# Merging the scores of two key blocks with a predicated copy, in the attention stage of a fused attention, mixture-of-experts and MLP kernel

## The chip, the core and the metric

The kernel runs on one core of a Trainium2 chip. The metric is the device time of one execution in microseconds (us). The core has five engines, each with an instruction stream of its own that runs in order: TensorE (PE in the profile; its weight loads are shown apart as PEld), VectorE (DVE), ScalarE (ACT), GpSimd (POOL) and SyncE (SP), which here only issues DMAs. The streams meet at semaphores: an instruction adds to one when it has finished, and another stream waits until it has reached a value.

## The reference

The batch is 4, there are 8 heads, 768 positions and 64 numbers per head. Attention keeps, for each position, the first 4 keys (the sinks) and the last 128 keys up to itself:

```python
scores = scale * np.matmul(q, k.transpose(0, 1, 3, 2))
keep = is_sink | in_window          # key < 4, or 0 <= query - key < 128
scores = np.where(keep, scores, -1e9)
a = np.exp(scores - max); a = a / (sum(a) + 1e-9)
attn = np.matmul(a, v)
x = attn as rows (3072, 512)
# mixture of experts: rows with x @ w_skip > 0 get the one expert of 8 with the largest gate logit
h = np.maximum(xc[mask] @ w1[e], 0); y[mask] = gate_w[mask, None] * (h @ w2[e]); out = x + y
# MLP on all rows
return np.maximum(x @ w_in, 0) ** 2 @ w_out
```

## The kernel before

Attention works on 24 tiles of 128 positions (`TILES`, six to a batch). A window of 128 keys that ends at the position itself lies in two blocks of keys: the tile's own block and the block before it. For a query in row r the own block gives keys 0 to r, and the block before gives the keys behind r: each column of the two blocks is wanted from one of them only, never from both. The first tile of a batch (`is_first`: tiles 0, 11, 17 and 23 in the order of work) has its own block alone. Each block is held with the 4 sinks in front, so it is `KB` = 132 columns wide.

For one tile i the stages are these. `scores(i, heads)` on PE multiplies queries and keys of a head into one of four PSUM banks (`SCORE_BANKS`), 264 columns wide (132 on a first tile); head n waits until the maximum of head n-4 has freed its bank. `maximum(i, h)` on DVE (L1190) reads a bank, adds a mask, scales and writes the scores and the row's negative maximum. `exps` on ACT (L667) makes the weights `prob`. `turn(i, k)` on PE (L897) turns the weights of a pair of heads k, four pieces of 128 x 128, and one `turn` for the sinks of all heads; `turned` on ACT (L680) copies them out of PSUM. `product(i, k)` on PE (L924) multiplies turned weights and values, own block and block before, into `oT_ps`. `take_output` (L1313, on DVE) copies `oT_ps` to `xT_a`, `logits` (L949) and `rows_back` (L935) on PE make the router's logits and turn the output back, `logits_back` turns the logits after DVE's `take_logits` (L1327), `normalise` on DVE (L1304) divides by the sum. DVE's `abreast` cuts the routing into pieces of tiny instructions (`choose`, `place`), one piece in front of each maximum. GpSimd splits the sink weights into two parts (`prob_sink`, L583 and L585) and scatters finished rows (L594).

The order on each engine is written out by hand, as a loop over steps i in which several tiles are at work. On PE step i is: turns 2, 3 and sinks of tile i-1; `scores(i, 4..7)`; four products of i-1; `logits` and `rows_back` of i-2; `turn(i, 0)`; ranks of i-3; `logits_back(i-2)`; `scores(i+1, 0..3)`; `turn(i, 1)`; the sink product of i-1. On DVE it is: `take_output(i-2)`; maxima 4 to 7 of tile i with routing pieces; sums; `take_logits` and `normalise` of i-2; reciprocals; maxima 0 to 3 of tile i+1, a routing piece in front of each. In steps 13 to 20 ACT also makes the upper half of the first expert's weights, and in steps 14 to 21 DVE the lower (L340, two a step).

Of the kernel before, what the change touches and what calls it, by code (L numbers as in the profile page):

```python
# [47 lines left out]
SINK = PAIRS  # L48
ITEMS = PAIRS + 1
# [26 lines left out]
def build(nc, n_sink, window, qT, kT, v, v_sink, w_route, weights, out):  # L76
# [10 lines left out]
    with ctx:  # L87
# [15 lines left out]
        masks = sb("masks", [P, 5, 2, KB], F32, big)  # L103
# [5 lines left out]
        score = sb("score", [P, 2, H, 2 * KB], F32, big)  # L109
        prob = sb("prob", [P, 2, H, 2 * KB], F32, big)  # L110
        prob_sink = sb("prob_sink", [P, 2, 2, H, NS], F32R, big)
        probT = sb("probT", [P, PAIRS, 4 * P], F32, big)
# [80 lines left out]
        bank = [ctx.enter_context(nc.psum_tensor(f"bank{n}", [P, 512], F32)) for n in range(8)]  # L193
# [20 lines left out]
        s_turn, s_turned, s_pv = sem("s_turn"), sem("s_turned"), sem("s_pv")  # L214
        s_xT, s_back = sem("s_xT"), sem("s_back")
# [34 lines left out]
        MASK_KINDS = ((1, 1, NS), (3, 1, 0), (4, 0, 0), (2, 0, NS))  # L250
        MASKS_MADE = (1, 3, 9, 5, 7)
# [45 lines left out]
        def mask_kind(i):  # L297

            return 0 if is_first(i) else {1: 2, 2: 4}[min(ORDER[i][1], 2)] - own_at(i)

        def width(i):

            return KB * len(blocks(i))
# [242 lines left out]
        def _(eng):  # L546
# [3 lines left out]
            def keep_up_to(part, first):  # L550

                eng.affine_select(out=part, in_=part, compare_op=ALU.is_ge, fill=out_of, base=-first, pattern=[[-1, P - first]], channel_multiplier=1)\
                   .then_inc(s_mask, 1)

            def keep_after(part, first):

                eng.affine_select(out=part, in_=part, compare_op=ALU.is_gt, fill=out_of, base=first, pattern=[[1, P - first]], channel_multiplier=-1)\
                   .then_inc(s_mask, 1)

            keep_up_to(masks[:, 0, 0, 2 * NS:KB], NS)  # L560
            eng.affine_select(out=ident[:, :], in_=ident[:, :], compare_op=ALU.not_equal, fill=1.0, base=0, pattern=[[-1, P]], channel_multiplier=1)\
               .then_inc(s_ident, 1)
            for kind, own, first in MASK_KINDS:
                keep_up_to(masks[:, kind, own, NS:KB], 0)
                keep_after(masks[:, kind, 1 - own, NS + first:KB], first)
# [11 lines left out]
            for i in range(TILES + 3):  # L577
                if i < TILES:
                    eng.wait_ge(s_exp, H * (i + 1))
                    if i >= 1:  # L580
                        eng.wait_ge(s_turn, ITEMS * i)
                    sinks = prob[:, i % 2, :, KB * own_at(i):KB * own_at(i) + NS].rearrange("p (v h) k -> p v h k", v=1).to_broadcast([P, 2, H, NS])
                    eng.tensor_copy(prob_sink[:, :, 0, :, :], sinks).then_inc(s_pshi, 1)  # L583
                    eng.wait_ge(s_pshi, i + 1)
                    eng.tensor_tensor(prob_sink[:, :, 1, :, :], sinks, prob_sink[:, :, 0, :, :].bitcast(F32), ALU.subtract).then_inc(s_psink, 1)  # L585
                j = i - 3
                if j < 0:
                    continue
                n = j % XR
                eng.wait_ge(s_slot, j + 1)  # L590
                if j == EARLY:
# [4 lines left out]
                   .then_inc(s_scatter[n], 16)  # L596

# [53 lines left out]
        def _(eng):  # L651
# [5 lines left out]
            def exps(i, heads):  # L657

                for h in heads:
# [7 lines left out]
                    eng.activation(prob[:, i % 2, h, 0:width(i)], score[:, i % 2, h, 0:width(i)], ACT.Exp, bias=neg_max[:, i % 2, h:h + 1],  # L667
                                   scale=-1.0, accum_out=row_sum[:, i % 2, h:h + 1]).then_inc(s_exp, 1)

            def turned(i, k):  # L670

                eng.wait_ge(s_turn, ITEMS * i + k + 1)
                if i >= 1:

                    eng.wait_ge(s_pv, ITEMS * (i - 1) + k + 1)
                if k == SINK:
                    eng.activation(sinkT[:, :], route_ps[:, SINKS:SINKS + P], ACT.Copy).then_inc(s_turned, 1)
                else:
                    cols = 2 * P * len(blocks(i))
                    eng.activation(probT[:, k, 0:cols], turn_ps[k % 2][:, 0:cols], ACT.Copy).then_inc(s_turned, 1)  # L680
# [21 lines left out]
            for i in range(TILES + 1):  # L702
# [9 lines left out]
                if bb:  # L712
                    turned(i - 1, 2)
                if a:
                    exps(i, (2,))
                if bb:
                    turned(i - 1, 3)
                    turned(i - 1, SINK)
                if a:
                    exps(i, (3,))  # L720
# [130 lines left out]
        def _(eng):  # L851
# [3 lines left out]
            def scores(i, heads):  # L855

                at = blocks(i)
                for h in heads:
# [10 lines left out]
                    eng.matmul(score_ps[n % SCORE_BANKS][:, 0:width(i)], q_in[rows, i % 3, h // 2, :], keys, start=True, stop=True).then_inc(s_score, 1)  # L869

            def turn(i, k):

                to = turn_ps[k % 2]
# [9 lines left out]
                else:  # L883
                    eng.wait_ge(s_exp, H * i + 2 * k + 2)

                    if k >= 2:
                        eng.wait_ge(s_turned, ITEMS * i + k - 1)
                    elif k == 0 and i >= 1:
                        eng.wait_ge(s_turned, ITEMS * i - 2)
                    elif k == 1 and i >= 2:  # L890
                        eng.wait_ge(s_x, i - 1)
                    elif k == 1 and i == 1:
                        eng.wait_ge(s_turned, ITEMS * i - 1)
                    u = 0
                    for half in range(2):
                        for at in range(len(blocks(i))):
                            ins = eng.transpose(to[:, u * P:(u + 1) * P], prob[:, i % 2, 2 * k + half, at * KB + NS:(at + 1) * KB], ident[:, :])  # L897
                            u += 1
                ins.then_inc(s_turn, 1)

            def product(i, k):
# [3 lines left out]
                eng.wait_ge(s_turned, ITEMS * i + k + 1)  # L905
                at = blocks(i)
# [674 lines left out]
```

## Time and profile before

| | us |
|---|---|
| median of 3 runs | 922.82 (922.46 to 923.65) |
| the profiled execution | 924.29 |
| its span, first to last instruction | 922.8 |
| of it attention, up to the drain of the last tile | about 190 |
| PE busy in the span | 899.4 (97%) |
| DVE, ACT, POOL busy | 473.3, 421.4, 81.7 |

"Busy" counts the time in which an engine has at least one instruction at work. The chain of waits is followed back from the last instruction: at each step to what released it, or to the instruction before it on its engine. A piece of it is therefore time that the end of the kernel has depended on. A timeline row gives start, duration, engine, line and operation, what it writes and reads, and in brackets how long the engine had been idle and what it then waited for.

### The profile page before, as it was taken

The numbers are of one execution on the slowest core, as the hardware profiler recorded it, in microseconds if no ns is written. First come the engines' busy times: TensorE is split into PE (matmuls) and PEld (weight loads), VectorE is DVE, ScalarE is ACT, GpSimd is POOL, SyncE is SP. The second block draws the span as 40 slices with busy tenths as digits, with TensorE's granted clock in tenths as the row PEclk, the third lists the DMA queues.
The fourth block names the chain that finished last, engine by engine and source line by source line (L and its number), as shares of the span: only waits on it lengthen the run. The fifth ranks groups of instructions, "written<-read, shape, count | busy, mean of one in ns | idle before, by whom it ended". The sixth has DMA issues, their size and how long they took to land.

```text
span 922.8 us, 16992 instructions
## 1 busy us (share of the span) xinstructions
PE 899.4 (97%) x5152; PEld 730.2 (79%) x5153; DVE 473.3 (51%) x1419; ACT 421.4 (46%) x970; POOL 81.7 (9%) x147
## 2 busy tenths in 40 slices
PE   7999999989999998999999999999999999999998
PEld 5778777757888886878888888888888888888886
DVE  5787899886776667764242224222422342243224
ACT  7888899835666666553132113221312231232123
POOL 3112121223111111100000000000000000000000
PEclk9999999999999999999999999999999999999999
DMA  5556675285667678740003002100400040004001
GB/s 200 170 160 201 225 239 173 71 296 186 240 248 250 245 245 311 242 106 0 1 36 57 1 1 67 24 0 0 91 0 0 0 91 0 0 0 91 0 0 45
DMA packets 87364, 99.52 MB, mean 108 GB/s; under 512 B 56093, under 2 KB 56221, under 8 KB 87312
## 3 DMA queue, kind: packets, MB, share of 16 engines
q1 hardware_dynamic: 81168, 83.34, 28.6%
q0 software_dynamic: 6000, 15.49, 4.9%
q8 instruction: 25, 0.41, 0.2%
q14 instruction: 27, 0.22, 0.1%
q10 hardware_dynamic: 144, 0.07, 0.0%
HBM read 77.72 MB, written 25.56 MB: 112 GB/s over the span
## 4 chain that ended last, share of the span: by engine, by line
PE 91%; issue 2%; ACT 2%; DMA 2%; DVE 2%; ACTq 1%; DVEq 0%; SPq 0%; POOLq 0%
PE bank L1128 28%; PE bank L1114 28%; PE bank L1029 7%; PE bank L1010 7%; PE bank L869 5%; PE bank L924 4%; PE bank L897 4%; PE bank L935 1%; PE bank L1018 1%; PE bank L949 1%; PE bank L917 1%; DMA w_raw<-in_weights 1%; PE bank L1002 1%; ACT prob L667 0%; DVE x_row L1304 0%
## 5 line engine op out<-in xcount | busy, mean ns | idle before, releaser
L1498 DVE TENSOR_TENSOR g<-relu_c 128x512 f32<-128x512 f32 x96 | 66.4, 692 | 340.7 <-ACT relu_c L812 340.7
L812 ACT ACTIVATE relu_c<-bank 128x512 f32<-128x512 f32 x96 | 57.4, 598 | 371.7 <-PE bank L1114 371.7
L1114 PE MATMUL bank<-x_hi,w_lo 128*128 128x512 f32 x384 | 149.5, 389 | 0.7 <-DVE x_lo L1485 0.7
L1128 PE MATMUL bank<-w_hi,g_lo 128*128 128x512 f32 x384 | 150.1, 391 | 0.0
L1128 PE MATMUL bank<-w_hi,g_hi 128*128 128x512 f32 x384 | 149.4, 389 | 0.0
L1128 PE MATMUL bank<-w_lo,g_hi 128*128 128x512 f32 x384 | 149.4, 389 | 0.0
L1114 PE MATMUL bank<-x_lo,w_hi 128*128 128x512 f32 x384 | 149.4, 389 | 0.0
L1114 PE MATMUL bank<-x_hi,w_hi 128*128 128x512 f32 x384 | 149.4, 389 | 0.0
L667 ACT ACTIVATE prob<-score,neg_max 128x264 f32<-128x264 f32 (+1 forms) x192 | 94.0, 496 | 15.2 <-DVE neg_max L1190 15.2
L1457 DVE TENSOR_TENSOR w_lo<-w_raw,w_hi x70 | 82.0, 1221 | 21.2 <-issue 13.3
L1128 PEld LDWEIGHTS bank<-w_hi,g_lo 128*128 128x128 f32 x384 | 72.1, 188 | 17.3 <-DVE g_lo L1505 2.5
L1114 PEld LDWEIGHTS bank<-x_hi,w_lo 128*128 128x128 f32 x384 | 72.1, 188 | 16.1 <-DVE x_lo L1485 1.2
L1128 PEld LDWEIGHTS bank<-w_hi,g_hi 128*128 128x128 f32 x384 | 72.1, 188 | 15.0
L1114 PEld LDWEIGHTS bank<-x_hi,w_hi 128*128 128x128 f32 x384 | 72.1, 188 | 15.0
L1114 PEld LDWEIGHTS bank<-x_lo,w_hi 128*128 128x128 f32 x384 | 72.1, 188 | 15.0
L1128 PEld LDWEIGHTS bank<-w_lo,g_hi 128*128 128x128 f32 x384 | 72.1, 188 | 14.8
L1190 DVE CUSTOM_DVE_ANT_0 score<-bank,masks 128x264 f32<-128x264 f32 (+1 forms) x192 | 74.4, 403 | 13.7 <-PE bank L869 5.3
L775 ACT ACTIVATE w_hi<-w_raw x70 | 69.5, 1050 | 18.7 <-DVE w_lo L1457 10.4
L1505 DVE TENSOR_TENSOR g_lo<-g,g_hi 128x512 fp32r<-128x512 f32 x96 | 65.6, 684 | 0.0
L821 ACT ACTIVATE g_hi<-g 128x512 fp32r<-128x512 f32 x96 | 60.0, 625 | 4.1 <-PE bank L1128 4.1
L869 PE MATMUL bank<-k_in,q_in 64*128 64x264 f32 (+1 forms) x384 | 54.9, 403 | 5.4 <-DMA k_in<-in_kT 5.4
L897 PE MATMUL bank<-ident,prob 128*128 128x128 f32 x352 | 56.0, 283 | 3.5 <-ACT probT L680 2.9
(149 smaller groups left out, 1280.3 us busy)
## 6 DMA issues: line engine op xcount, KB each, us to landing
w_raw<-in_weights SPq DMA_DIRECT2D x80, 512.0 KB, 4.9
k_in<-in_kT SPq DMA_DIRECT2D x24, 264.0 KB
q_in<-in_qT SPq DMA_DIRECT2D x24, 256.0 KB, 3.4
v_in<-in_v SPq DMA_DIRECT2D x24, 256.0 KB
x_rows<-x_row SPq DMA_DIRECT2D x24, 256.0 KB, 3.3
x_row<-x_rows SPq DMA_DIRECT2D x96, 64.0 KB, 2.4
out<-w_raw SPq DMA_DIRECT2D x12, 512.0 KB, 2.9
x_res<-routed POOLq DMA_DIRECT2D x15, 260.0 KB, 3.4
```

The source lines that it names most:

```text
L667: eng.activation(prob[:, i % 2, h, 0:width(i)], score[:, i % 2, h, 0:width(i)], ACT.Exp, bias=neg_max[:, i % 2, h:h + 1], scale=-1.0, accu ...
L775: eng.activation(w_hi[1 - slot][:, f, :], w_raw[:, f, :], ACT.Copy).then_inc(s_whi, 1)
L869: eng.matmul(score_ps[n % SCORE_BANKS][:, 0:width(i)], q_in[rows, i % 3, h // 2, :], keys, start=True, stop=True).then_inc(s_score, 1)
L897: ins = eng.transpose(to[:, u * P:(u + 1) * P], prob[:, i % 2, 2 * k + half, at * KB + NS:(at + 1) * KB], ident[:, :])
L1010: ins = eng.matmul(h_ps[half][:, :], x[:, c, :], w[:, c, cols], start=(c == 0 and k == 0), stop=(c == DC - 1 and k == 2))
L1029: ins = eng.matmul(y_ps[:, :], h[:, c // 4, at], w[:, DC + c // 2, cols], start=(c == 0 and k == 0), stop=(c == FC - 1 and k == 2))
L1114: ins = eng.matmul(hc_ps[f % 2][:, :], w[f // UNIT][:, f % UNIT, wcols], x[:, c, :], start=(c == 0 and n == 0), stop=(c == DC - 1 and n == 2))
L1128: ins = eng.matmul(yc_ps[s][:, :], gg[:, f % 2, s * P:(s + 1) * P], w[f // UNIT][:, f % UNIT, DM:CH], start=(f == 0 and n == 0), stop=(f = ...
L1190: eng.tensor_tensor_reduce(score[:, i % 2, h, 0:width(i)], score_ps[n % SCORE_BANKS][:, 0:width(i)], masks[:, mask_kind(i), 0:len(blocks(i ...
L1457: eng.tensor_tensor(w_lo[1 - slot][:, f, :], w_raw[:, f, :], w_hi[1 - slot][:, f, :].bitcast(F32), ALU.subtract).then_inc(s_wlo, 1)
L1498: eng.tensor_tensor(g[:, f % 2, :], relu_c[:, f % 2, :], relu_c[:, f % 2, :], ALU.mult).then_inc(s_cg, 1)
L1505: eng.tensor_tensor(g_lo[:, f % 2, :], g[:, f % 2, :], g_hi[:, f % 2, :].bitcast(F32), ALU.subtract).then_inc(s_cglo, 1)
```

## The change

Two scores of a column are never both wanted, so one instruction on DVE, `merge(i, k)`, copies the block before over the own block in PSUM where the column lies behind the query, for four heads (all four banks) at once. From there on a head has 132 columns instead of 264: the maximum, the exponential and the scores' and weights' buffers. PE turns four pieces for four heads instead of eight, and ACT copies them out in one instruction per four heads. The products still need own block and block before apart, so GpSimd splits the turned weights with two selections per four heads (`split`): one writes `probT_own`, the other clears `probT` in place. `take_output` moves from DVE to ACT within the loop. PE's order changes: the turn of heads 4 to 7 now lies at the start of the next step, and the products are two, the second behind `rows_back`. GpSimd's scatter of a tile moves one turn of its loop later. `quad` is the four score banks as one tensor. The masks are fewer, and first tiles are neither merged nor split.

```diff
 # GpSimd
+def split(i, k):
+    if is_first(i): return
+    eng.wait_ge(s_turned, ITEMS * i + k + 1)
+    eng.affine_select(out=probT_own[:, k, :, :], in_=probT[:, k, :, :], compare_op=ALU.is_ge, fill=0.0, base=0,
+                      pattern=[[0, QUAD], [1, P]], channel_multiplier=-1).then_inc(s_split, 1)
+    eng.affine_select(out=probT[:, k, :, :], in_=probT[:, k, :, :], compare_op=ALU.is_gt, fill=0.0, base=0,
+                      pattern=[[0, QUAD], [-1, P]], channel_multiplier=1).then_inc(s_split, 1)
-for i in range(TILES + 3):
+for i in range(TILES + 4):
+    if 1 <= i <= TILES: split(i - 1, 1)
+    if i >= 4: scatter(i - 4)
     ...
+        split(i, 0)
 # ScalarE, step i
-    exps(i, (1,)); turned(i - 1, 2); exps(i, (2,)); turned(i - 1, 3); turned(i - 1, SINK); exps(i, (3,))
+    exps(i, (1,)); turned(i - 1, SINK); take_output(i - 2); exps(i, (2, 3))
 # TensorE
-    eng.wait_ge(s_turned, ITEMS * i + k + 1)
+    if k == SINK or is_first(i): eng.wait_ge(s_turned, ITEMS * i + k + 1)
+    else: eng.wait_ge(s_split, SPLITS * others(i) + 2 * k + 2)
     ...
-                    turn(i - 1, 2)
-                    turn(i - 1, 3)
+                    turn(i - 1, 1)
                     turn(i - 1, SINK)
                 if a:
                     scores(i, (4, 5, 6, 7))
                 if bb:
-                    for k in range(PAIRS):
-                        product(i - 1, k)
+                    product(i - 1, 0)
                 if c:
                     logits(i - 2)
                     rows_back(i - 2)
+                if bb:
+                    product(i - 1, 1)
                 if a:
                     turn(i, 0)
     ...
-                if a:
-                    turn(i, 1)
 # VectorE
+def merge(i, k):
+    eng.wait_ge(s_score, H * i + QUAD * (k + 1))
+    if is_first(i): return
+    own, other = (slice(at * KB + NS, at * KB + KB) for at in (own_at(i), 1 - own_at(i)))
+    eng.copy_predicated(quad[:, :, own], later_keys[:, :, :].bitcast(I32), quad[:, :, other]).then_inc(s_merged, 1)
 def maximum(i, h):
-    eng.wait_ge(s_score, n + 1)
+    if h % QUAD == 0 and not is_first(i):
+        eng.wait_ge(s_merged, QUADS * others(i) + h // QUAD + 1)
     ...
-                if c:
-                    take_output(i - 2)
+                if a:
+                    merge(i, 1)
     ...
                 if i + 1 < TILES:
+                    merge(i + 1, 0)
                     for h in range(4):
                         next(routing, None)
                         maximum(i + 1, h)
```

## Rows read from the trace of the kernel before

**Rows 1.** Busy time in a stretch: PE, PEld, DVE, ACT, POOL, granted clock, DMA share, GB/s

```profile
100.00:120.00 20.00, 20.00 (x207) 15.70 (x209) 17.71 (x105) 18.90 (x62) 4.53 (x9) 1.00 0.70 234
```

**Rows 2.** Chain that ended last, one step: start, us, engine and line

```profile
103.18 1.09 PE bank L869 x8
104.27 1.90 PE bank L924 x32
106.17 0.36 PE bank L949 x8
106.52 0.59 PE bank L935 x4
...
107.75 1.09 PE bank L869 x8
108.84 0.59 PE bank L897 x4
...
109.83 1.01 PE bank L897 x8
...
110.94 1.09 PE bank L869 x8
```

**Rows 3.** Same chain: the turn of the sinks in steps 3 and 23

```profile
26.07 0.11 PE bank L882
...
180.26 0.11 PE bank L882
```

**Rows 4.** Groups by line and form: count, busy us, mean ns, idle before

```profile
L667 ACT ACTIVATE prob<-score,neg_max 128x264 f32<-128x264 f32 x160 | 81.3, 515 | 12.1 <-DVE neg_max L1190 12.1
L1190 DVE CUSTOM_DVE_ANT_0 score<-bank,masks 128x264 f32<-128x264 f32 x160 | 65.9, 426 | 10.0 <-PE bank L869 5.1 <-DVE slot_i L1264 3.4
L680 ACT ACTIVATE probT<-bank 128x512 f32<-128x512 f32 x80 | 47.3, 591 | 4.7 <-PE bank L897 4.7
L1313 DVE COPY xT_a<-bank 128x512 f32<-128x512 f32 x24 | 16.5, 686 | 0.2
L1190 DVE CUSTOM_DVE_ANT_0 score<-bank,masks 128x132 f32<-128x132 f32 x32 | 8.5, 288 | 3.7 <-issue 2.8 <-DVE slot_i L1264 0.6 <-PE bank L869 0.3
L552 POOL TENSOR_SCALAR_AFFINE_SELECT masks<-masks 128x128 f32<-128x128 f32 x4 | 1.1, 282 | 0.0
```

**Rows 5.** Chain, step 1: four scores on PE

```profile
12.61 1.09 PE bank L869 x8
```

**Rows 6.** Timeline of DVE, step 1: the first maximum of those four heads

```profile
13.29 0.43 DVE L1190 CUSTOM_DVE_ANT_0 score<-bank,masks 128x264 f32<-128x264 f32 x1 [1.64 <-PE bank L869]
```

**Rows 7.** Timeline of DVE: a routing piece in front of the first maximum

```profile
100.16 0.18 DVE L1199 TENSOR_TENSOR head_logit<-bank,recip 128x72 f32<-128x72 f32 x1
...
100.41 0.14 DVE L1243 TENSOR_SCALAR expsum_eps<-expsum 128x1 f32<-128x1 f32 x1
```

**Rows 8.** Timeline of DVE, step 18: first and fourth maximum, then two copies

```profile
139.75 0.42 DVE L1190 CUSTOM_DVE_ANT_0 score<-bank,masks 128x264 f32<-128x264 f32 x1
...
141.87 0.43 DVE L1190 CUSTOM_DVE_ANT_0 score<-bank,masks 128x264 f32<-128x264 f32 x1 [0.20 <-DVE slot_i L1264]
...
142.22 0.69 DVE L1313 COPY xT_a<-bank 128x512 f32<-128x512 f32 x1
142.83 0.68 DVE L340 TENSOR_TENSOR w_lo<-w_raw,w_hi 128x512 fp32r<-128x512 f32 x1
```

**Rows 9.** Chain, step 18: the products behind scores that waited for those maxima

```profile
143.07 1.08 PE bank L924 x16
```

**Rows 10.** Timeline of DVE: maxima 4 to 7 with routing, first and next

```profile
103.77 0.15 DVE L1222 TENSOR_REDUCE best<-cand 128x1 f32<-128x8 f32 x1
...
105.54 0.17 DVE L1290 TENSOR_SCALAR sum_eps<-row_sum 128x8 f32<-128x8 f32 x1
```

**Rows 11.** Busy time by stretch as in Rows 1: the drain of attention

```profile
184.00:193.00 9.00, 6.15 (x68) 4.50 (x66) 7.02 (x40) 2.65 (x8) 1.32 (x2) 1.00 0.95 322
193.00:196.00 3.00, 2.72 (x9) 1.70 (x10) 1.93 (x12) 0.39 (x2) 0.98 (x1) 0.52 1.03 416
```

More of the change, by code:

```diff
@@ L297, in mask_kind, with others @@
         def mask_kind(i):
-            return 0 if is_first(i) else {1: 2, 2: 4}[min(ORDER[i][1], 2)] - own_at(i)
-        def width(i):
-            return KB * len(blocks(i))
+            return min(ORDER[i][1], LATER)
+        def others(i):
+            return sum(not is_first(n) for n in range(i))
         def step_flags(i):
@@ L883, in turn @@
                 else:
[L884 to L889, printed above, removed]
+                    eng.wait_ge(s_exp, H * i + QUAD * (k + 1))
+                    if k == 0 and i >= 1:
+                        eng.wait_ge(s_turned, ITEMS * (i - 1) + 1)
                     elif k == 1 and i >= 2:
@@ L892, in turn @@
                     elif k == 1 and i == 1:
[L893 to L898, printed above, removed]
+                        eng.wait_ge(s_turned, 2)
+                    for u in range(QUAD):
+                        ins = eng.transpose(to[:, u * P:(u + 1) * P], prob[:, i % 2, QUAD * k + u, NS:KB], ident[:, :])
                 ins.then_inc(s_turn, 1)
             def product(i, k):
-                eng.wait_ge(s_turned, ITEMS * i + k + 1)
-                at = blocks(i)
+                if k == SINK or is_first(i):
+                    eng.wait_ge(s_turned, ITEMS * i + k + 1)
+                else:
+                    eng.wait_ge(s_split, SPLITS * others(i) + 2 * k + 2)
                 if k == 0:
@@ L919, in product @@
                 else:
-                    for n, ring in enumerate(at):
-                        for half in range(2):
-                            h = 2 * k + half
-                            u = half * len(at) + n
-                            ins = eng.matmul(oT_ps[half * D:(half + 1) * D, k * P:(k + 1) * P], v_in[:, ring, h * D:(h + 1) * D],
-                                             probT[:, k, u * P:(u + 1) * P],
-                                             start=(k == 0 and n == 0), stop=False, skip_group_check=True)
+                    own = own_load(i) % RING, probT if is_first(i) else probT_own
+                    parts = [own] if is_first(i) else [own, (before_load(i) % RING, probT)]
+                    for p in range(QUAD // 2):
+                        for n, (ring, part) in enumerate(parts):
+                            for half in range(2):
+                                u = 2 * p + half
+                                h = QUAD * k + u
+                                ins = eng.matmul(oT_ps[half * D:(half + 1) * D, h // 2 * P:(h // 2 + 1) * P], v_in[:, ring, h * D:(h + 1) * D],
+                                                 part[:, k, u, :], start=(k == 0 and p == 0 and n == 0), stop=False, skip_group_check=True)
                 ins.then_inc(s_pv, 1)
@@ L1074, in expert @@
                     tile(n, slot, parts)
-            turn(TILES - 1, 2)
-            turn(TILES - 1, 3)
+            turn(TILES - 1, 1)
             turn(TILES - 1, SINK)
-            for k in range(PAIRS):
+            for k in range(QUADS):
                 product(TILES - 1, k)
```

116 lines of the change are left out of this document (64 added, 52 removed).

## The prediction, made before the changed kernel was run

> **What bounds the kernel now.** I read the busy table by stretch first. In attention PE is busy for all of 20 us, ACT for 18.90 and DVE for 17.71, at full granted clock [rows 1]: three engines near their limit, so the table doesn't say which one a change is worth something on. The chain of waits does: through most of attention it runs piece after piece on PE with no wait between, and the step repeats after 7.76 us (the scores of heads 4 to 7 at 103.18 and at 110.94) [rows 2]. From the sinks' turn in step 3 to that in step 23 twenty steps take 154.2 us, 7.71 each [rows 3]. Nothing behind attention is touched but the places in the code and 8 buffers, so the forecast is a sum over these steps.
>
> **PE's work.** The change takes away eight of the sixteen turns, the piece of 1.01 us [rows 2]. All other matmuls stay: scores are still 264 wide on PE, and the products still need own block and block before. Alone, PE would need 7.76 - 1.01 = 6.75 us a step. The question is whether it is kept fed.
>
> **The new round trip.** Call T0 the end of the scores of heads 0 to 3 of a tile, T1 the end of those of heads 4 to 7. Both groups use the same four banks. Before, the first maximum began as soon as the first pair of heads had landed. Now the merge waits for all four heads, and the first maximum for the merge; and it stands ahead of the routing piece on DVE, which used to run while the scores were under way. Between T0 and T1 PE has only the sink product, four turns and the sinks' turn: 110.94 - 108.84 = 2.10, less the 1.01 that goes: 1.09 us; before the change the 2.10 just covered the maxima. From T0 to T1 the steps are now:
> - PE to DVE: a group took 1.09 us [rows 5], and its first maximum came 13.29 - 12.61 = 0.68 us after its start [rows 6]. That is the first pair, half the group; the last pair is 0.545 later, 0.14 behind the group's end.
> - The merge: no row shows a predicated copy, nor DVE writing PSUM. The nearest is the copy of 128x512 out of PSUM, 686 ns [rows 4], 0.61 from its start to the next instruction's [rows 8]. It has as many columns; I take 0.61. Below it I see no gain, since it reads a mask besides; above, twice as much, 1.22.
> - The routing piece in front of the first maximum: 0.25 from its first to its last start [rows 7], with an estimated 0.06 for the last 0.31.
> - The four maxima with the other routing pieces, and the last score. In step 18 of before PE did wait for these maxima: the first started at 139.75, the fourth at 141.87 [rows 8], and the work behind the last score at 143.07 [rows 9]. That is 3.32 us. Each maximum gets shorter by 426 - 288 = 138 ns [rows 4], four by 0.55: 2.77.
>
> The sum is 0.14 + 0.61 + 0.31 + 2.77 = 3.83 us. PE has 1.09 of other work and 1.09 of scores to put into it, so it stands still for 1.65 us.
>
> **The rest of the step** holds the same instructions as before, in another order: from 104.27 (products) to 108.84 (end of the next scores) 4.57 us [rows 2]. The second merge and maxima 4 to 7 lie under this: 0.14 + 0.61 + (105.54 - 103.77 - 0.55 = 1.22) [rows 10] is 2.0, and the next scores are asked for after 3.5. A step is then 3.83 + 4.57 = 8.40 us, against 7.71.
>
> **The other parts.** ACT loses two of four copies of 591 ns and 132 of 264 columns of eight exponentials of 515 ns [rows 4]; it gains the output copy. It is not in the round trip, but PE's products at T1 wait for that copy now: first maximum, an exponential, a copy, another exponential, the sinks and the output copy end about 3.6 us behind T0, so just hidden under 3.83; if that cover goes it costs some tenths a step. DVE loses 8 x 0.138 and the output copy, 0.61, and gains two merges, 1.22: about 0.5 less, and it waits for PE anyway. GpSimd gains four selections a step. One over 128 columns took 282 ns [rows 4]; over 512 it lies between that and four times as much, 1.13. I take the upper end, as the work is by column. Four are 4.5 us, on top of 4.53 / 20 x 7.76 = 1.76 [rows 1], of a step of 8.4. The splits of heads 4 to 7 begin at T0 + 2.5 and end by 4.8; their product is asked for at T1 + 0.95 + 0.36 + 0.59 [rows 2], T0 + 5.7. So they are hidden, and would bind from about 1.6 us each. The scatter moves one turn of GpSimd's loop, behind two waiting splits; the row buffer that it frees is wanted two steps later, and at the end of attention it can delay the first expert tile's load once, by two selections at most, 2.3 us; I cost it at nothing, for the drain is full of other waits.
>
> In steps 14 to 21 DVE also makes the weights' lower halves, 0.61 each as spaced [rows 8]. Then `take_logits` ends at T1 + 0.14 + 0.61 + 0.61 + 1.22 + 0.10 + 0.61 + 0.35 = 3.64, and PE wants its result about 0.3 earlier: 0.3 more in each of these eight steps.
>
> **The sum.** Twenty steps at 8.40 are 168.0. Add 8 x 0.3 = 2.4. Where the batch changes I take off, by estimate, 0.44 three times (narrow scores), 0.95 once (half the products) and 0.83 twice (no merge): 3.9. That is 166.5 against 154.2: +12.3. Steps 1 and 2 have little or no routing, and there the 1.01 comes through about once: -1.0. Net +11.3 us. The profiled execution took 924.29 (span 922.8 and 1.5 around it), so it would go to 935.6; the median of the runs was 922.82, 1.5 lower, and goes to **934.1 us**.
>
> **Rival: PE stays the bound.** Then a step is 6.75 and twenty save 20 us: 903. For that the round trip must be 2.18 or less. Already merge and four bare maxima, 0.14 + 0.61 + 4 x 0.29 = 1.9, and the last score, at least a quarter of 1.09, come to that. The point at which the kernel stops losing is a round trip of 3.83 - 11.3 / 20 = 3.26, so if some 0.6 us of the routing vanished beside the maxima, of about 1.3 (0.31, and what the 2.12 holds beside three maxima, 0.85 to 1.0). For it speaks that these instructions overlap a little; against it that each piece waits for the one before, and that the 3.32 is measured with the overlap in it. About 912, chance 0.08; another 0.06 for no change, 921 to 924.7.
>
> **Rival: GpSimd holds up DVE.** The second pair of splits begins at T0 + 2.5, and just then DVE runs the last routing piece in front of the fourth maximum. If the two engines got in each other's way there, a routing instruction would wait for up to one selection, 0.28 to 1.13; at 0.6 this is 12 us more, 946. The Trainium skill says that it is so (SBUF — State Buffer, "Who interferes with whom"): a DVE instruction with two inputs in SBUF and a GpSimd instruction that reads SBUF exclude each other for the length of one; two instructions of that piece, `cand` and `slot_i`, have two such inputs. No row here shows it, as GpSimd is busy for a quarter of the time [rows 1] and elsewhere. A merge of 1.22 would give the same size: +12. Together 0.28.
>
> **Rival: the clock falls.** In the drain PE was busy for 6.15 of 9 us, 68%, and then the granted clock was 0.52, the lower level (1.2 GHz) [rows 11]. A step of 6.75 in 8.40 is 80%. If half the steps ran their 4.57 at the lower clock, they would take 10 x 4.57 = 46 us more: 980. Chance 0.06, as the stall is broken up by four scores.
>
> **How the numbers follow.** The forecast as summed, 925 to 940, has 0.52. Faster by over 0.2% (about what a measurement of this kernel can tell from no change) has 0.08, within 0.2% 0.06, slower 0.52 + 0.28 + 0.06 = 0.86. The range goes from 924 to 952: it takes in the forecast and the rival with GpSimd or a dear merge, and leaves out the faster case, most of no change, and the clock.
>
> **What would show it.** In the profile after, PE should be idle for some 1.6 us a step in front of the scores of heads 4 to 7, the wait ending on DVE's negative maximum, and the chain should go through merge, maxima and routing pieces. The piece of turns should be gone, the products as long as before. The merge should take about 0.69 us, a selection under 1.13. I am wrong if PE's chain is still unbroken, if a step is under 7.7 us, or if PE waits in front of the products for GpSimd or ACT instead.

## The result and the profile after

The changed kernel takes 947.63 us (946.52 to 948.08), the kernel before beside it 923.15: a ratio of 1.0264, 95% interval 1.0246 to 1.0282. That is 24.5 us slower where 11.3 had been forecast; the sign and the range held, but the forecast was less than half of what came. The profiled spans differ by 22.7 us (945.5 and 922.8).

The busy line of the page after (engine, busy us, share of the span, instructions):

```profile
PE 918.5 (97%) x4992; PEld 727.0 (77%) x4993; DVE 464.3 (49%) x1427; ACT 396.5 (42%) x944; POOL 130.4 (14%) x221
```

PE looks full, and is not. The ends of matmuls are modelled in the profile, and the modelled lengths of the scores cover most of the waits between their banks: from 115.01 to 118.77 us PE counts as busy for 3.65 of 3.76 us. The chain shows the wait. One step of the changed kernel, to be read against [rows 2] (start us, us, what):

```profile
115.01 0.02 issue
115.03 0.70 DVE quad L1205
115.73 0.09 DVE head_logit L1225
...
116.01 0.26 DVE score L1216
...
117.70 0.30 DVE score L1216
...
118.06 0.71 PE quad L891 x2
118.77 1.02 PE bank L946 x16
119.79 0.35 PE bank L970 x8
120.15 0.59 PE bank L956 x4
120.74 1.02 PE bank L946 x16
121.76 0.59 PE bank L915 x4
...
122.55 1.14 PE quad L891 x8
123.69 0.02 issue
123.71 0.70 DVE quad L1205
```

The chain leaves PE for 3 us in an ordinary step: T0 is at 115.01, then merge, routing pieces and maxima on DVE, and only the last head's scores bring it back; T1 is at 118.77. The step is 8.68 us long, where [rows 2] has 7.76.

What the parts cost, from the groups by form up to the first expert tile (busy us, mean ns of one | idle before):

```profile
L1205 DVE COPY_PREDICATED quad<-later_keys,quad 128x512 f32<-128x512 int32 x40 | 27.8, 696 | 46.7 <-PE quad L891 46.7
L1216 DVE CUSTOM_DVE_ANT_0 score<-quad,masks 128x132 f32<-128x132 f32 x192 | 52.3, 287 | 9.1 <-DVE slot_i L1290 4.0 <-issue 3.8 <-PE quad L891 0.9
L685 ACT ACTIVATE prob<-score,neg_max 128x132 f32<-128x132 f32 x192 | 75.7, 397 | 56.1 <-DVE neg_max L1216 54.7 <-issue 1.5
L585 POOL TENSOR_SCALAR_AFFINE_SELECT probT_own<-probT 128x512 f32<-128x512 f32 x40 | 25.6, 640 | 43.4 <-ACT probT L697 43.4
```

The merge is the 0.69 that was named, a maximum 287 ns against the 426 of [rows 4], and a selection 0.64, well under the 1.13 taken for it. ACT, at 18.90 of 20 us before [rows 1], now has 56 us of idle time in front of its exponentials, nearly all of it waiting for DVE's maxima.

Where the 22.7 us of the span lie, by the start of the sinks' turn in each tile (tiles 2 and 22 are at 25.91 and 180.10 before, at 30.34 and 202.16 after; the first expert matmul at 192.90 and 216.68):

| stretch | forecast | measured |
|---|---|---|
| to tile 2 | -1.0 | +4.4 |
| tile 2 to tile 22, twenty steps | +12.3 | +17.6 |
| tile 22 to the first expert matmul | 0 | +1.7 |
| behind it | 0 | -1.1 |

### The profile page after: what moved, and what is told of

Read it like the earlier page. It is cut to its first block, busy times and chain, and to the rows that moved or that the text cites. A ratio compares the mean times of both kernels' runs of the same rounds, so it can differ in the third digit from the quotient of the medians.

```text
span 945.5 us, 16614 instructions
## 1 busy us (share of the span) xinstructions
PE 918.5 (97%) x4992; PEld 727.0 (77%) x4993; DVE 464.3 (49%) x1427; ACT 396.5 (42%) x944; POOL 130.4 (14%) x221
## 4 chain that ended last, share of the span: by engine, by line
PE 86%; DVE 7%; issue 3%; DMA 1%; ACT 1%; ACTq 1%; DVEq 0%; SPq 0%; POOLq 0%
PE bank L1146 28%; PE quad L1132 28%; PE bank L1048 7%; PE quad L1029 7%; PE bank L946 5%; PE quad L891 5%; DVE score L1216 2%; PE bank L915 2%; DVE quad L1205 1%; PE bank L956 1%; PE bank L970 1%; PE quad L1021 1%; PE quad L1037 1%; DMA w_raw<-in_weights 1%; PE bank L1037 1%
## 5 line engine op out<-in xcount | busy, mean ns | idle before, releaser
L834 ACT ACTIVATE relu_c<-quad 128x512 f32<-128x512 f32 x96 | 57.4, 598 | 371.6 <-PE quad L1132 371.6
L1132 PE MATMUL quad<-x_hi,w_lo 128*128 128x512 f32 x384 | 149.5, 389 | 0.7 <-DVE x_lo L1513 0.7
L1132 PE MATMUL quad<-x_hi,w_hi 128*128 128x512 f32 x384 | 149.4, 389 | 0.0
L1132 PE MATMUL quad<-x_lo,w_hi 128*128 128x512 f32 x384 | 149.4, 389 | 0.0
L685 ACT ACTIVATE prob<-score,neg_max 128x132 f32<-128x132 f32 x192 | 75.7, 397 | 56.1 <-DVE neg_max L1216 54.7
L891 PE MATMUL quad<-k_in,q_in 64*128 64x264 f32 (+1 forms) x384 | 79.7, 420 | 9.7 <-DMA k_in<-in_kT 5.5
L1132 PEld LDWEIGHTS quad<-x_hi,w_lo 128*128 128x128 f32 x384 | 72.1, 188 | 16.1 <-DVE x_lo L1513 1.1
L1132 PEld LDWEIGHTS quad<-x_hi,w_hi 128*128 128x128 f32 x384 | 72.1, 188 | 15.0
L1132 PEld LDWEIGHTS quad<-x_lo,w_hi 128*128 128x128 f32 x384 | 72.1, 188 | 14.9
L797 ACT ACTIVATE w_hi<-w_raw x70 | 69.6, 1051 | 17.6 <-DVE w_lo L1485 9.4
L1216 DVE CUSTOM_DVE_ANT_0 score<-quad,masks 128x132 f32<-128x132 f32 x192 | 52.3, 287 | 9.1 <-DVE slot_i L1290 4.0
```

Of the source, the lines that this page charges most:

```text
L685: eng.activation(prob[:, i % 2, h, :], score[:, i % 2, h, :], ACT.Exp, bias=neg_max[:, i % 2, h:h + 1], scale=-1.0, accum_out=row_sum[:, i ...
L797: eng.activation(w_hi[1 - slot][:, f, :], w_raw[:, f, :], ACT.Copy).then_inc(s_whi, 1)
L891: eng.matmul(score_ps[n % SCORE_BANKS][:, 0:KB * len(at)], q_in[rows, i % 3, h // 2, :], keys, start=True, stop=True).then_inc(s_score, 1)
L1132: ins = eng.matmul(hc_ps[f % 2][:, :], w[f // UNIT][:, f % UNIT, wcols], x[:, c, :], start=(c == 0 and n == 0), stop=(c == DC - 1 and n == 2))
L1216: eng.tensor_tensor_reduce(score[:, i % 2, h, :], score_ps[h % QUAD][:, own_at(i) * KB:own_at(i) * KB + KB], masks[:, mask_kind(i), :], -S ...
```

## The experiments

Theory: in each step PE stands still in a round trip through DVE over the four banks, as forecast; on top of it come single terms of the sum that were mis-sized. Rivals: GpSimd's selections hold up DVE or the products; the clock. Two more questions came from the table: the start, and the seams between kinds of work on PE. The table gives every kernel tried. The ratio is to the kernel before as run beside each, whose median lay between 923.15 and 925.02, so medians of two rows compare to within some 2 us. The columns behind it are read from the start of the sinks' turns in the one profile of each kernel: where tile 2 begins, the step from tile 6 to 7 (an ordinary one), from 10 to 11 (tile 11 is a batch's first tile), and from 19 to 20 (DVE makes weights' halves); then the first expert matmul.

| kernel | median us | ratio to before (95%) | tile 2 | 6-7 | 10-11 | 19-20 | expert |
|---|---|---|---|---|---|---|---|
| before | 923.15 | | 25.91 | 7.76 | 7.50 | 7.76 | 192.90 |
| after | 947.63 | 1.0246-1.0282 | 30.34 | 8.67 | 10.30 | 8.75 | 216.68 |
| e1_product_later | 933.69 | 1.0066-1.0126 | 28.10 | 7.65 | 7.65 | 8.76 | 201.58 |
| e2_piece_first | 944.69 | 1.0192-1.0248 | 29.68 | 8.60 | 9.90 | 8.67 | 214.59 |
| e3_both | 932.07 | 1.0056-1.0111 | 28.01 | 7.66 | 7.66 | 8.69 | 201.25 |
| e4_no_splits | 949.74 | 1.0250-1.0314 | 27.86 | 8.66 | 8.20 | 8.74 | 211.08 |
| e6_copy_twice | 980.50 | 1.0566-1.0641 | 33.01 | 9.41 | 9.48 | 10.22 | 252.21 |
| e7_start | 943.80 | 1.0183-1.0252 | 27.07 | 8.67 | 8.75 | 8.75 | 211.84 |
| e8_pieces_behind | 941.53 | 1.0150-1.0221 | 28.28 | 8.45 | 8.20 | 8.45 | 208.34 |
| e9_pieces_act | 930.42 | 1.0055-1.0103 | 29.16 | 7.61 | 7.16 | 8.32 | 196.02 |
| e10_act | 943.68 | 1.0197-1.0250 | 27.52 | 8.67 | 8.31 | 8.75 | 211.00 |
| e11_dense_start | 944.77 | 1.0199-1.0256 | 26.69 | 8.67 | 8.76 | 8.75 | 211.45 |
| e12_sparse_start | 946.12 | 1.0206-1.0279 | 29.06 | 8.67 | 8.75 | 8.75 | 216.88 |
| e13_seam | 944.85 | 1.0186-1.0235 | 30.37 | 8.63 | 8.16 | 8.75 | 213.48 |
| v4_all | 923.24 | 0.9976-1.0011 | 28.11 | 7.12 | 6.53 | 8.30 | 191.72 |
| v5_halves | 917.86 | 0.9910-0.9945 | 26.47 | 7.12 | 6.53 | 7.68 | 183.82 |
| v6_start | 917.05 | 0.9896-0.9952 | 26.67 | 7.12 | 6.53 | 7.67 | 184.17 |

### Work for the round trip

```
                     rows_back(i - 2)
-                if bb:
-                    product(i - 1, 1)
...
                 if bb:
+                    product(i - 1, 1)
                     product(i - 1, SINK)
```

> The products of heads 4 to 7 of the tile before are moved behind the scores of heads 0 to 3 of the next tile, on PE alone; all else is the changed kernel. Theory (round trip through DVE over the four banks): the piece of 1.02 us moves out of the chain behind the second scores (4.92 to 3.90 us) into the stall, where PE stands still for about 1.6 us; the round trip stays at 3.76, a full step goes from 8.67 to about 7.7 us and the time by about 20 us, to 925 to 932. Rival (GpSimd's selections hold up DVE or the products) and rival (the clock): the amount of each engine's work is the same, so a step stays at about 8.6 and the time at 944 to 950.

An ordinary step fell from 8.67 to 7.65, the 1.02 of the moved piece to a hundredth; the rivals, by which it would have stayed at about 8.6, are out for ordinary steps. The time, 933.69, missed the 925 to 932: most steps in which DVE makes weights' halves stayed near 8.76. Their chain (start us, us, what) and the end of their queue on DVE (start us, us, instruction):

```profile
167.35 0.44 PE bank L915 x4
167.78 0.94 issue
168.73 0.17 PE bank L985
```
```profile
167.74 0.69 DVE L348 TENSOR_TENSOR w_lo<-w_raw,w_hi 128x512 fp32r<-128x512 f32 x1
168.34 0.28 DVE L1353 COPY lgT<-bank 128x128 f32<-128x128 f32 x1
```

PE stands 0.94 us in front of the ranks, which wait for the logits' copy, and that copy is queued on DVE behind a weights' half. The round trip is not the only loop there.

### The parts of the round trip

e6_copy_twice makes each merge twice, the second behind the first:

```
+                eng.copy_predicated(quad[:, :, own], later_keys[:, :, :].bitcast(I32), quad[:, :, other]).then_inc(s_again, 1)
+                eng.wait_ge(s_again, QUADS * others(i) + k + 1)
                 eng.copy_predicated(quad[:, :, own], later_keys[:, :, :].bitcast(I32), quad[:, :, other]).then_inc(s_merged, 1)
```

> Each merge of the changed kernel is made twice, the second copy behind the end of the first (the second changes nothing in the scores). Theory (round trip through DVE): the copy in front of heads 0 to 3 lies in the round trip, 0.70 us and up to 0.17 for the wait behind it, in twenty steps: 14 to 17 us more, 961 to 966; the copy in front of heads 4 to 7 stays hidden. Rival (the time is lost where PE's products wait for GpSimd or ACT, or at the clock; DVE has some 2.9 us of slack in a step): 0 to 4 us more, 947 to 952.

The ordinary step rose by 0.74, from 8.67 to 9.41: the merge ahead of heads 0 to 3 lies wholly on the path. The time rose by 33, twice what was expected. In the steps with weights' halves both merges count, by the size of the rise (10.22 against 8.75), and six steps took 10.9 to 12.5, with the granted clock down in five of them. A stretch in one of these (us, PE busy, PEld, DVE, ACT, POOL, granted clock, DMA share, GB/s):

```profile
86.00:88.00 2.00, 2.00 (x16) 1.45 (x16) 1.31 (x3) 0.78 (x6) 1.01 (x1) 0.50 0.17 26
```

0.50 is the lower level, 1.2 GHz; from 82 to 84 us, at 1.00, PE had been busy for 1.22 of 2.00 us. So the rival with the clock is real, at a longer stall than the change makes.

```
+                    next(routing, None)
                     merge(i + 1, 0)
                     for h in range(4):
-                        next(routing, None)
+                        if h:
+                            next(routing, None)
                         maximum(i + 1, h)
```

> On DVE the first routing piece is put back in front of the first merge of a tile, so that it runs while the scores of heads 0 to 3 are under way. Theory (round trip): about 0.3 us leaves the round trip in each of some twenty steps: 940 to 943. Rival (GpSimd) and rival (clock): 946 to 949.

The step fell by 0.07, not 0.3. With the piece gone, DVE stands idle for 0.17 us between the merge and the first maximum, which waits for the merge's end; the routing piece had been running in that gap (timeline of DVE, idle time and its releaser in brackets):

```profile
62.75 0.29 DVE L1216 CUSTOM_DVE_ANT_0 score<-quad,masks 128x132 f32<-128x132 f32 x1 [0.17 <-DVE quad L1205]
```

e3_both has both edits:

> Both edits: the products of heads 4 to 7 behind the next tile's first scores on PE, and the first routing piece ahead of the first merge on DVE. Theory (round trip): 3.45 us of round trip hold 1.09 + 1.02 + 1.14 = 3.25 us of PE's work, 3.90 stand outside: a step of about 7.35 us, and the time near 919 to 925, about that of the kernel before. Rivals: above 940.

7.66 and 932.07, no less than e1 alone and above what was expected: something else ends as late as DVE's loop. The next two kernels name it.

```
                     merge(i + 1, 0)
+                    next(routing, None)
                     for h in range(4):
-                        next(routing, None)
                         maximum(i + 1, h)
+                    for _ in range(3):
+                        next(routing, None)
```

> On DVE the second, third and fourth routing pieces stand behind the four maxima of heads 0 to 3 instead of between them; all else is the changed kernel. Theory (round trip): these pieces lie in the round trip, about 0.75 us: a full step goes from 8.67 to about 7.9 us, a little less in the steps with the weights' halves, and the time to 931 to 937. Rival (routing instructions overlap the maxima or PE's other work anyway) and rival (GpSimd, clock): 944 to 949.

Only 0.22 a step. The products at T1 now wait for ACT's output copy, and no longer for DVE (timelines of PE and ACT, idle time and its releaser in brackets):

```profile
73.59 0.44 PE L946 MATMUL bank<-probT_own,v_in 128*64 128x128 f32 x4 [0.77 <-ACT xT_a L705]
```
```profile
72.86 0.59 ACT L705 ACTIVATE xT_a<-bank 128x512 f32<-128x512 f32 x1
```

The products begin 3.47 us behind T0 (70.12), where the prediction has "about 3.6" for the end of that copy. In e3's chain it is the same copy (67.49 to 68.09, its products at 68.23): there the moved product stands ahead of PE's turn of heads 4 to 7, and so of all that ACT does behind it. e10 makes that copy earlier on ACT, in the changed kernel, and e9 does so in e8:

```
                     exps(i, (0,))
+                if a and c:
+                    take_output(i - 2)
                 if bb:
                     turned(i - 1, 1)
...
-                if a and c:
-                    take_output(i - 2)
```

> The changed kernel with the output copy ahead of the copy of the second turned weights on ACT, nothing else. Theory (DVE's loop of 3.76 us ends last in the changed kernel, ACT's is hidden under it): no change, 945 to 949. Rival (the products' wait for the output copy is what limits the changed kernel): 0.2 us and more a step, 943 or below.

> The changed kernel with the second to fourth routing pieces behind the four maxima on DVE and, besides, the output copy on ACT ahead of the copy of the second turned weights. Theory (two loops of nearly the same length between the two groups of scores: DVE's with merge and maxima, 3.76 us, and ACT's with exponential, two copies and the output copy, about 3.5): with both shortened the round trip is DVE's without the pieces, about 3.0, and a full step 7.9 to 8.0 us where DVE makes no halves of the weights, 8.2 to 8.5 where it does: 931 to 937. Rival (what is left behind the moved pieces is not ACT's loop): a step stays at 8.45 and the time at 940 to 943.

Alone the move changes no ordinary step (8.67), as expected; the time, 943.68, still lies under the 945 to 949. In the profile that gain comes from tiles 0 to 2 (2.8 us) and from the step to tile 11 (2.0), below. With the routing pieces out of the way it takes 0.84 off the step, from 8.45 to 7.61, more than expected: the round trip comes to 2.70 and not 3.0 (7.61 less 4.91 from the products to the end of the next scores). So there are two loops between the two groups of scores, 3.76 and about 3.5 us long, and the second hides what is taken off the first. In e9 neither ends last. The sinks' turn on PE waits for `carry`, an instruction of the first routing piece, which stands behind the merge (chain of e9, T0 at 66.08, T1 at 68.78):

```profile
67.01 0.08 DVE carry L1262
...
67.14 0.33 PE bank L904
67.47 1.31 PE quad L891 x8
```

### GpSimd

```
-                if is_first(i):
-                    return
...
+                return
...
-                if k == SINK or is_first(i):
+                if True:
                     eng.wait_ge(s_turned, ITEMS * i + k + 1)
...
-                    own = own_load(i) % RING, probT if is_first(i) else probT_own
+                    own = own_load(i) % RING, probT
```

> GpSimd's selections are left out, and both products of a head use the unsplit weights (so the weights of both blocks are applied to both blocks' values); waits, copies and matmuls are otherwise those of the changed kernel. Theory (round trip; the selections cost only at the three first tiles, where one of them lies on DVE's routing instruction, 0.5 us and the lowered clock behind it): full steps stay at 8.67, the time falls by 3 to 6 us, 941 to 945. Rival (GpSimd holds up DVE or the products in every step): a step is shorter by 0.5 us and more, 937 or below.

Its ordinary steps are those of the changed kernel, 8.66: the selections cost nothing there. The step to tile 11 falls from 10.30 to 8.20, and the expert stage begins 5.6 us earlier. The whole time says nothing here: behind attention this kernel took 735.9 us against 728.8, with 7.7 us of PE waiting for ACT behind the experts' first layer against 3.4. Unsplit weights give another output of attention, and by argument another routing; that it is the routing was not tried. In the step to tile 11 of the changed kernel (start us, us, instruction):

```profile
98.85 0.68 DVE L1246 SCALAR_TENSOR_TENSOR cand<-logit,top,falling 128x8 f32<-128x8 f32 x1
98.88 0.64 POOL L585 TENSOR_SCALAR_AFFINE_SELECT probT_own<-probT 128x512 f32<-128x512 f32 x1 [0.72 <-ACT probT L697]
100.16 0.58 PE L891 MATMUL quad<-k_in,q_in 64*128 64x132 f32 x2 [0.76 <-DVE neg_max L1216]
```

`cand`, 0.22 us otherwise, takes 0.68 and ends with the selection, to 0.01 us. The Trainium skill (SBUF — State Buffer, "Who interferes with whom") says that a DVE instruction with two inputs in SBUF contends with a GpSimd instruction that reads SBUF, and the row agrees. It happens where a first tile without a merge brings DVE's routing forward onto the selections, in three steps (98.85, 151.24, 203.16); in e7 `slot_i`, the other instruction that the prediction names, takes 0.59 there. What follows is dearer than the wait (windows as above, granted clock behind POOL's count):

```profile
98.00:100.00 2.00, 1.41 (x9) 0.89 (x7) 1.80 (x14) 2.00 (x8) 1.28 (x3) 1.00 0.59 227
100.00:102.00 2.00, 1.84 (x14) 1.62 (x16) 1.32 (x15) 1.74 (x11) 1.12 (x2) 0.61 0.41 15
102.00:104.00 2.00, 2.00 (x20) 1.17 (x16) 0.44 (x4) 0.85 (x5) 0.55 (x2) 0.54 0.72 274
```

PE's busy share falls, and then the clock is near its lower level for almost 4 us. Such a dip does not always bring it; e7 has the same collision, and its clock stays at 1.00:

```profile
96.00:98.00 2.00, 1.27 (x18) 1.02 (x18) 1.22 (x10) 1.83 (x9) 1.72 (x3) 1.00 0.09 35
```

The same step with the collision and without that fall took 8.75 (e7, e11, e12), without the collision 8.16 to 8.31 (e4, e8, e10, e13): 0.5 for the collision, 1.55 for the clock.

### The start

Tiles 0 to 2 cost 5.4 us more than forecast. PE's timeline after (start us, us, instructions):

```profile
10.10 2.13 PE L891 MATMUL quad<-k_in,q_in 64*128 64x264 f32 x8
...
16.13 1.98 PE L946 MATMUL bank<-probT,v_in 128*64 128x128 f32 x16
...
18.83 1.16 PE L891 MATMUL quad<-k_in,q_in 64*128 64x264 f32 x8
```

Eight scores take 2.13 us at first and 1.16 later: half speed until about 18 us, though the granted clock of these rows reads 1.00; in the kernel before they take 1.16 from 12.54 on. e7 and e11 fill PE's gaps with turns of the identity, into a bank not yet in use; e12 makes one gap longer:

```
+            def fill(n):
+                for u in range(n):
+                    eng.transpose(oT_ps[:, u % QUAD * P:(u % QUAD + 1) * P], ident[:, :], ident[:, :])
...
             scores(0, (0, 1, 2, 3))
+            eng.wait_ge(s_ident, 1)
+            fill(4)
...
+                if i == 1:
+                    fill(2)
...
+                if i == 0:
+                    fill(3)
                 if a:
                     turn(i, 0)
```

> Nine extra turns of the identity, into the bank that the products use later, stand in PE's idle places of the first steps: four behind the first scores, three ahead of the first turns, two in the second step. Theory on the start (PE's work runs at half speed until about 18 us, in the kernel before until 12.5, because it has gaps at 6 to 10 us): with the gaps filled the full speed comes earlier, the sinks' turn of tile 1 comes 1.5 to 3 us earlier, 943 to 946. Rival (the late start is only the first round trips over the banks, or the speed does not hang on the gaps): 947 to 949.

e11 has `fill(8)` ahead of the first scores and `fill(4)` at the three places:

> The changed kernel with more extra turns of the identity than e7_start: eight ahead of the first scores, while PE waits for the first keys, and four in each of the three later gaps of the first steps. Theory (PE gets its full speed once its work has no gaps): PE's work is at full speed from about 8 us, in the profile and in every timed run, and the sinks' turn of tile 1 comes at about 18 instead of 20.88: 942 to 945, the runs close together. Rival (the moment at which the speed rises does not hang on PE's gaps): full speed at 13 or 18 us as in the kernels without extra turns, 944 to 948.

And e12:

```
+                if i == 0:
+                    eng.wait_ge(s_exp, QUAD)
                 if a:
                     scores(i, (4, 5, 6, 7))
```

> The changed kernel with one more wait in the first step: the second four scores of the first tile wait for the exponentials of the first four, so that PE stands still for some 1 to 2 us more there. Theory (full speed hangs on work without gaps): full speed at 18 us or later, the sinks' turn of tile 1 at 21 to 24; 947 to 951. Rival (it does not): the delay of 1 to 2 us in the first step is partly made up, full speed may come at 13 us; 944 to 948.

PE's timeline in e11, and then in e12:

```profile
9.48 1.16 PE L891 MATMUL quad<-k_in,q_in 64*128 64x264 f32 x8
```
```profile
8.66 1.25 PE L891 MATMUL quad<-k_in,q_in 64*128 64x132 f32 x8 [2.21 <-ACT prob L685]
10.89 2.13 PE L891 MATMUL quad<-k_in,q_in 64*128 64x264 f32 x8
14.57 1.44 PE L891 MATMUL quad<-k_in,q_in 64*128 64x264 f32 x8 [0.77 <-DVE neg_max L1218]
```

With the gaps filled full speed comes before 9.5 us (e11), and tile 2 begins 3.3 (e7) and 3.7 us (e11) earlier than after; the medians lie 3.8 and 2.9 us lower, but in the profiles 1.55 of the gain is the step to tile 11 at full clock. But e12, with 2.21 us of idle time, is at full speed by 14.57, earlier than the changed kernel with its shorter gaps: the expectation of 18 or later fell. (Its first expert matmul is as late as after's, since the lowered clock behind a collision cost it 3.1 us in the step to tile 17, 11.86 against 8.78 in e7, with the granted clock at 0.50.)

So gaps alone don't set the moment; e4, e10 and v5, with the gaps of the changed kernel, have full speed by 13 (the sinks' turn of tile 0 takes 0.27 us there, at 12.65 to 12.96, and 0.42 in the changed kernel, at 13.07). What makes 13 or 18 of it stays open. The Trainium skill (TensorE: Matmul & The Clock Gate, "Part 1: The HAM clock gate") says that the change to the fast clock varies from run to run, as the check that grants it runs free of the kernel. That would let kernels with like gaps differ, but each has one profile here, so no run shows it.

The half speed accounts for some 3 us of the 5.4. The rest stands in e11 too: its tile 2 still begins 0.8 behind the kernel before, where 1.0 ahead had been forecast. The profile after has two waits there. In the step to tile 2 DVE's loop has no routing, is shorter than ACT's, and covers it no more; PE waits for the output copy (timeline of PE):

```profile
23.43 0.44 PE L946 MATMUL bank<-probT_own,v_in 128*64 128x128 f32 x4 [0.78 <-ACT xT_a L705]
```

e10, with that copy earlier, takes 8.38 for this step against 9.2 in e7 and e11 and 9.45 in the changed kernel. And the sinks' turn of tile 2 itself waits 1.00 us for DVE's routing, which the step behind it gives back (7.43 for the ordinary 8.67).

### The seams

```
-                if bb:
-                    product(i - 1, 1)
                 if a:
                     turn(i, 0)
+                if bb:
+                    product(i - 1, 1)
```

> On PE of the changed kernel the four turns of heads 0 to 3 stand ahead of the products of heads 4 to 7 instead of behind them, so behind the turns of the output. Theory (the piece from the products to the next scores is 0.35 us longer than forecast because some of PE's instructions take longer behind another kind: the turns 0.59 behind the products, 0.44 behind turns): the turns take 0.44, a full step 8.5 to 8.55 instead of 8.67, the time 943 to 946. Rival (the 0.15 moves to the next seam): 8.67 and 946 to 949.

The turns took 0.44 as expected, and the ranks behind the products now 0.11 instead of 0.01; the step fell by 0.04. Most of the gain went to the next seam, as the rival says. Most of the 2.8 us of the median are not from the seam: the step to tile 11 had no collision (8.16 for 10.30).

### A version that beats both

v4_all joins e3, e8 and the early output copy; v5_halves also moves DVE's two halves of the weights, one ahead of the second merge, the other behind the reciprocals:

```
-                if a:
-                    merge(i, 1)
                 if i >= TILES - UNIT - 2 and i < TILES - 2:
                     lower_half(eng, i - (TILES - UNIT - 2), 0)
+                if a:
+                    merge(i, 1)
...
                     reciprocals(i - 1)
+                if i >= TILES - UNIT - 2 and i < TILES - 2:
+                    lower_half(eng, i - (TILES - UNIT - 2), 1)
```

> Four moves of order in the changed kernel: on PE the products of heads 4 to 7 behind the next tile's first scores; on DVE the first routing piece ahead of the first merge and the three others behind the four maxima; on ACT the output copy ahead of the copy of the second turned weights. Theory (round trip): it comes to about 2.9 us, holds 2.18 us of other work and the scores of 1.09, so PE does not stand still; 3.27 + 3.90 is a step of about 7.2 us where DVE makes no weights' halves, and 7.6 to 8.3 where it does: 912 to 922, below the kernel before. Rivals (GpSimd's feed of the products, the clock): 930 or above.

> The four moves of order of v4_all and two more on DVE: of the two lower halves of the weights in a step the first stands ahead of the second merge, the second behind the normalisation and the reciprocals, so that PE's turns of the logits do not wait behind them. Theory (in these steps DVE's queue in front of the logits' copy sets the step, 8.30 us): such a step falls to 7.6 to 8.0, and the step of 10.26 with its lowered clock goes too: 914 to 920. Rival (DVE has more to do in these steps than the step is long, wherever it stands): 8.2 to 8.3 us, 921 to 924.

> v5_halves with the nine extra turns of the identity of e7_start in PE's gaps of the first steps. Theory on the start: another 2 to 4 us less than v5_halves, 911 to 917. Rival (the start is hidden behind the loads or is given back): the same as v5_halves.

v4 equals the kernel before, and misses the 912 to 922: its ordinary step is 7.12, but the steps with halves take 8.30 and one of them 10.26. They fell to 7.68 in v5, which is 0.55 to 0.90% faster than the kernel before. v6's extra turns add nothing that can be told from v5, whose full speed had come by 12.7 anyway. A step of v5 (chain):

```profile
62.43 1.09 PE quad L891 x8
63.52 1.02 PE bank L946 x16
64.55 0.35 PE bank L970 x8
64.90 0.59 PE bank L956 x4
65.49 0.44 PE bank L915 x4
65.92 0.16 PE bank L985
66.08 0.03 PE bank L986
66.10 0.17 PE bank L976
66.27 1.09 PE quad L891 x8
67.36 1.02 PE bank L946 x16
68.39 0.59 PE bank L936 x4
68.98 0.46 PE bank L915 x4
69.44 0.11 PE bank L904
```

In such a step PE is never released by another engine, and it takes 7.12: this is the rival "PE stays the bound", reached by order alone.

## Why the prediction was right in sign and short in size

The spans differ by 22.7 us where 11.3 had been forecast. Of the 11.4 that were missing 5.4 lie in steps 1 and 2, 5.3 in the twenty steps and 1.7 in the drain, with 1.1 given back behind it. The stall was found where it was forecast; what failed is the pricing of the reordered piece behind it and, more, of the irregular steps: the start and the changes of batch.

- **The round trip** is right, nearly to the hundredth: 3.83 forecast, 3.76 measured (PE idle 3.76 - 1.09 - 1.14 = 1.53 for 1.65), with 0.70 for the merge and 2.76 (116.01 to 118.77) for maxima, routing and the last score against 2.77. e1 and e6 show that it sets the step. Only the routing piece at 0.31 was no cost of its own: 0.07 in e2.
- **T1 to the next T0** is the mis-sized term of the step. What "holds the same instructions as before, in another order" was costed at 4.57 and measured 4.92 (118.77 to 123.69): two half products are 2.04 where the whole ones of [rows 2] are 1.90, the turns behind them 0.59 for 0.44, the scores 1.14 for 1.09. e13 shows that such seams move rather than go. The same error stands in "alone, PE would need 6.75": with PE never waiting, v5's step is 7.12, so that eight turns fewer freed 0.64 and not 1.01.
- **The twenty steps** gave +17.6 for +12.3. Of the excess of 5.3 the steps to tiles 11 and 17 hold 3.6: forecast as 8.40 - 0.83 = 7.57 and 8.70 - 0.83 = 7.87, measured 10.30 and 8.79. The steps at a batch's change were taken as gains, and the rival with GpSimd struck in them alone; it had been priced in every step and given 0.28 together with a dear merge. e4 shows the place; the lowered clock behind one of the collisions, 1.55, is the largest part of the 3.6. The other eighteen steps hold the remaining 1.7: ordinary ones 8.67 for 8.40, those with DVE's halves 8.75 for 8.70, and against that the step behind tile 2, 7.43.
- **Steps 1 and 2**, -1.0, is the term with the wrong sign: +4.4. That routing is missing there doesn't take away the merge and the wait for four heads, and it uncovers ACT's loop (0.78 of waiting); PE's slow start was not in the sum, and e7 and e11 give back 3 us and more of it.
- **The drain**, costed at nothing, took 1.7 more. 1.2 of it is the step from tile 22 to 23 (7.15 for 5.95), and some 0.5 of that the third collision (6.68 in e4, 6.64 in e13, which do not have it). The rest, and the 1.1 that the expert stage gave back, stay open; behind the first expert matmul all kernels but e4 lie between 727.8 and 732.7, before at 729.9 and after at 728.8.
- **ACT** was right for an ordinary step: its loop, with products that can begin at 3.47, lies just under 3.76, and e8 shows the price when the cover goes. In the step to tile 2 it went in the changed kernel itself. **GpSimd's length** was overestimated by 0.5 us a selection, without effect.
- **PE stays the bound** could not hold in the order as changed; **the clock** fell in one step of the changed kernel's attention, not in half of them, and in e6, with 0.74 more of stall a step, in several.

## What to carry to other kernels

Where two engines hand the same few buffers to and fro, write down every loop between the two uses with its length, and put independent work of the waiting engine into the longest: here moving one product gave 14 us, and moving what ended second-last gave an ordinary step nothing until the last had moved. Don't price a reordered piece by its old neighbours, and don't count the irregular steps (first tiles, the start) as discounts: look at which instructions of the other engines come to lie beside them there.

## What the runs showed of the hardware

- A predicated copy of 128x512 within PSUM takes 0.696 us, as a plain copy out of PSUM does (686 ns, [rows 4]), and an instruction behind it that doesn't wait for it starts 0.09 us ahead of its end. What waits for its end starts later: e6's second copy 0.03 us behind it, e2's first maximum mostly 0.17. Why these two differ stays open.
- A selection on GpSimd took 282 ns over 128 columns [rows 4] and 640 over 512: 2.3 times for four times the columns.
- One wait of 0.46 us on DVE (`cand` at 0.68 for 0.22), let through to PE, was followed by nearly 4 us near the lower clock, 1.55 us more in that step; in e12 it was 3.1. In e7 and e11 such waits were not followed by it.
- At the start PE's work ran at about half speed until some moment between 8 and 18 us, by kernel, while the granted clock read 1.00.
